# Low part of g on GpSimd, key grams one slot earlier, one-piece inverse steps and gate weights in parts, in an attention and two-MoE kernel

## What is computed

```python
k_n = k / (np.linalg.norm(k, axis=-1, keepdims=True) + 1e-06)
for t in range(S):
    y[:, :, t] = einsum('bhd,bhde->bhe', q[:, :, t], state)
    v_old = einsum('bhde,bhd->bhe', state, k_n[:, :, t])
    state = state + beta[:, :, t] * outer(k_n[:, :, t], v[:, :, t] - v_old)
h = x @ w_in                       # x: y as 3072 x 384
x2 = maximum(0.01 * h, h) @ w_out
logits = x2 @ w_gate + modality_bias[modality_id]
e = argmax(logits)                 # gate_w: softmax(logits)[e]
out = gate_w * (maximum(x2 @ w1[e], 0) @ w2[e])
```

## Time and profile before

| | |
|---|---|
| median of 3 runs | 1023.89 us (1022.36 to 1029.06) |
| profiled execution | 1023.64 us |
| its span | 1021.9 us |
| mean granted clock of PE | 0.951 |
| PE, DVE, ACT, POOL busy | 932.1, 554.3, 351.7, 87.8 us |

### The profile page before, as it was taken

One profiled execution on the slowest core, in us unless ns is written; L12 is line 12 of the kernel. 1 busy time (PEld: TensorE's weight loads), 2 busy tenths in 40 slices (PEclk: granted clock), 3 DMA queues, 4 the chain that ended last, 5 costly groups with the idle time before them and its releaser, 6 DMA issues.

```text
span 1021.9 us, 26857 instructions
## 1 busy us (share of the span) xinstructions
PE 932.1 (91%) x10524; PEld 832.1 (81%) x10525; DVE 554.3 (54%) x1577; ACT 351.7 (34%) x608; POOL 87.8 (9%) x100
## 2 busy tenths in 40 slices
PE   4897699999999999999999999999988999999972
PEld 4896588878888889888888888888877898888962
DVE  5936795389626983498428862334562333333341
ACT  4255234542534343433444242332511222212230
POOL 1000000000020000100010001001021212212211
PEclk8659899999999999999999999999998999999996
DMA  9803181235223440345143411317132111111122
GB/s 161 283 2 73 36 159 57 72 87 88 56 47 89 95 80 26 87 103 94 26 87 81 86 30 29 98 38 202 40 112 99 46 31 46 38 39 46 31 78 70
DMA packets 147923, 77.91 MB, mean 76 GB/s; under 512 B 112112, under 2 KB 143856, under 8 KB 147440
## 3 DMA queue, kind: packets, MB, share of 16 engines
q1 hardware_dynamic: 143728, 66.98, 27.9%
q0 software_dynamic: 4096, 9.48, 3.0%
HBM read 59.30 MB, written 13.21 MB: 71 GB/s over the span
## 4 chain that ended last, share of the span: by engine, by line
PE 73%; DVE 12%; DMA 4%; ACT 3%; issue 3%; SPq 3%; DVEq 0%; POOL 0%; ACTq 0%; POOLq 0%
PE bank L486 16%; PE bank L471 14%; PE bank L567 10%; PE bank L542 9%; PE bank L430 3%; PE bank L457 2%; PE bank L415 2%; PE bank L454 2%; PE bank L362 2%; SPq L737 2%; PE bank L552 2%; DVE inv_t L1264 2%; DVE inv_tmp L1258 2%; PE bank L504 2%; PE bank L383 1%
## 5 line engine op out<-in xcount | busy, mean ns | idle before, releaser
L486 PE MATMUL bank<-wo_hi,g_hi 128*128 128x392 f32 x384 | 138.8, 361 | 8.3 <-DVE g_lo L1338 5.4
L1011 ACT ACTIVATE g_raw<-bank 128x512 f32<-128x512 f32 x96 | 57.3, 597 | 227.4 <-PE bank L471 225.0
L1333 DVE SCALAR_TENSOR_TENSOR g_raw<-g_raw 128x512 f32<-128x512 f32 x96 | 66.2, 690 | 123.6 <-ACT g_raw L1011 122.8
L471 PE MATMUL bank<-x_hi,wi_hi 128*128 128x512 f32 x288 | 118.2, 411 | 16.1 <-DVE x_lo L1329 12.6
L486 PE MATMUL bank<-wo_hi,g_lo 128*128 128x392 f32 x384 | 132.0, 344 | 0.0
L486 PE MATMUL bank<-wo_lo,g_hi 128*128 128x392 f32 x384 | 131.8, 343 | 0.0
L471 PE MATMUL bank<-x_hi,wi_lo 128*128 128x512 f32 x288 | 113.7, 395 | 0.0
L471 PE MATMUL bank<-x_lo,wi_hi 128*128 128x512 f32 x288 | 113.6, 394 | 0.0
L1018 ACT ACTIVATE g_hi<-g_raw 128x512 fp32r<-128x512 f32 x96 | 60.6, 631 | 105.7 <-DVE g_raw L1333 102.6
L1338 DVE TENSOR_TENSOR g_lo<-g_raw,g_hi 128x512 fp32r<-128x512 f32 x96 | 66.1, 689 | 41.8 <-ACT g_hi L1018 40.9
L486 PEld LDWEIGHTS bank<-wo_hi,g_hi 128*128 128x128 f32 x384 | 72.7, 189 | 14.2 <-issue 6.8
(11 more groups left out here) (211 smaller groups left out, 1664.2 us busy)
## 6 DMA issues: line engine op xcount, KB each, us to landing
wo_lo<-wo_lo_d SPq DMA_DIRECT2D x80, 196.0 KB
w_raw<-in_moe_w SPq DMA_DIRECT2D x6, 1536.0 KB, 8.4
x_rows<-stage SPq DMA_DIRECT2D x6, 770.0 KB
kq_in_rows<-in_k SPq DMA_DIRECT2D x6, 768.0 KB, 5.4
k_raw<-in_k SPq DMA_DIRECT2D x24, 192.0 KB, 4.6
vals<-in_v SPq DMA_DIRECT2D x24, 192.0 KB, 4.7
kq_in_rows<-in_q SPq DMA_DIRECT2D x6, 768.0 KB, 7.8
x_raw<-y_t SPq DMA_DIRECT2D x36, 96.0 KB, 2.5
```

Source lines behind the costliest of these rows:

```text
L471: mm = pe.matmul(bank[0][:], a[:, m, P * f:P * f + P], x[:, m, :], start=(m == 0 and x is x_hi and a is wi_hi), stop=(m == KT - 1 and a is ...
L486: mm = pe.matmul(acc[i][:, 0:DX], g[f % 2][:, P * i:P * i + P], w, start=(f == 0 and k == 0), stop=(f == FT - 1 and k == 2))
L1011: act.activation(g_raw[f % 2][:], bank[0][:], ACT.Copy).then_inc(s.hs_ev, 1)
L1333: dve.scalar_tensor_tensor(out=g_raw[f % 2][:], in0=g_raw[f % 2][:], scalar=0.01, in1=g_raw[f % 2][:], op0=ALU.mult, op1=ALU.max).then_inc ...
```

## The change

- `g_lo` is made by POOL instead of DVE in slices f = 0 to 5 and 13 to 15 of a tile (not the very first slice, not in the last tile, and 13 to 15 not in the last two): the slots that hold inverse steps. Two semaphores count the two makers.
- The key transposes all stand at f = 8, the four grams at f = 9 and 10, `norm` at 11, `scale_gram` and the first steps at 12: one slot sooner. The steps end at f = 3 instead of 4.
- An inverse step is one product and one addition instead of two of each; each waits for the one before it.
- The gate weights are made in parts 0 to 8 at (-1, 4), 9 and 10 at (-1, 12), and 11 to 15 at (-1, 13), ahead of the first `up`. The buffers `wo_t` move from x_raw's place to one that overlaps no_token, stage and g_hi; ACT waits for `list_out` before its first copy, and SP no longer waits for the gate products before it loads x. `rest_gate_weights` moves behind `split_x(0)`.
- POOL walks the slots too; its clearing of `inv_t` stands at f = 5, its scatters at f = 9.

```diff
-INV_AT = {13: (0, 5), 14: (5, 9), 15: (9, 13), 0: (13, 17), 1: (17, 21), 2: (21, 25), 3: (25, 30), 4: (30, INV)}
+INV_AT = {12: (0, 4), 13: (4, 9), 14: (9, 12), 15: (12, 16), 0: (16, 20), 1: (20, 24), 2: (24, 28), 3: (28, INV)}
...
-        wo_t = [same_place(f"wo_t{i}", [P, KT, P], sb.at + 4 * DM * i, F32) for i in range(2)]
...
+        wo_t = [same_place(f"wo_t{i}", [P, KT, P], sb.at + at, F32) for i, at in enumerate((2560, 6144))]
...
+        def g_on_pool(n, f):
+
+            return n <= TT - 2 and f < 6 and n + f > 0 or n <= TT - 3 and f >= 13
...
-                pe.wait_ge(s.g_rdy, j + 1)
+                pe.wait_ge(*g_count(n, f))
...
                 if n == -1 and f == 13:
+                    gate_weights(11, FT)
                     up(0, 0)
...
                 if n == -1 and f == 4:
-                    gate_weights()
+                    gate_weights(0, 9)
+                if n == -1 and f == 12:
+                    gate_weights(9, 11)
...
                     if f == 8:
-                        keys_t(n + 2, 0)
-                        keys_t(n + 2, 1)
+                        for m in range(4):
+                            keys_t(n + 2, m)
                     if f == 9:
-                        keys_t(n + 2, 2)
-                        keys_t(n + 2, 3)
+                        gram_k(n + 2, 0)
+                        gram_k(n + 2, 1)
                     if f == 10:
-                        gram_k(n + 2, 1)
-                    if f == 11:
+                        gram_k(n + 2, 2)
                         gram_k(n + 2, 3)
...
-                if n == -1 and f == 10:
-                    sp.wait_ge(s.wx_mm, FT)
...
+            def rest_g(n, f):
+                pool.wait_ge(s.gh_ev, FT * n + f + 1)
+                pool.tensor_tensor(g_lo[f % 2][:], g_raw[f % 2][:], g_hi[f % 2][:].bitcast(F32), ALU.subtract).then_inc(s.g_rdy_p, 1)
...
-            def gate_weights():
-                for f in range(FT):
+            def gate_weights(first, end):
+                if first == 0:
+                    act.wait_ge(s.list_out, 16)
+                for f in range(first, end):
...
+                made = counted(dve.tensor_tensor(
+                    tmp, inv_a[:, j, j + 1:].unsqueeze(2).broadcast_to([P, rows, cols]),
+                    inv_t[:, j, 0:cols].unsqueeze(1).broadcast_to([P, rows, cols]), ALU.mult))
+                dve.wait_ge(s.inv_ch, made)
+                rows_t = inv_t[:, j + 1:, 0:cols]
+                counted(dve.tensor_tensor(rows_t, rows_t, tmp, ALU.add))
```

More of the change, by code:

```diff
@@ L170, in build @@
         inv_t = sb("inv_t", [P, BLK, BLK])
-        inv_tmp = [sb(f"inv_tmp{i}", [P, BLK * BLK // 4]) for i in range(2)]
+        inv_tmp = sb("inv_tmp", [P, BLK * BLK // 4])
         u_sb = sb("u_sb", [P, GROUPS, HD])
@@ L328, in is_set, with g_count @@
             return 0 <= t < SETS
+        def g_on_pool(n, f):
+            return n <= TT - 2 and f < 6 and n + f > 0 or n <= TT - 3 and f >= 13
+        def g_count(n, f):
+            pool = g_on_pool(n, f)
+            done = sum(1 for m in range(n + 1) for e in range(f + 1 if m == n else FT) if g_on_pool(m, e) == pool)
+            return (s.g_rdy_p if pool else s.g_rdy_d), done
         def slots():
@@ L488, in down @@
                 mm.then_inc(s.l2_mm, 1)
-            def gate_weights():
-                pe.wait_ge(s.misc_in, 16 * 6)
-                for f in range(FT + 1):
-                    if f < FT:
+            def gate_weights(first, end):
+                if first == 0:
+                    pe.wait_ge(s.misc_in, 16 * 6)
+                for f in range(first, end + 1):
+                    if f < end:
                         if f % 4 == 0:
@@ L500, in gate_weights @@
                         mm.then_inc(s.wt_mm, 1)
-                    if f:
+                    if f > first:
                         pe.wait_ge(s.wt_ev, f)
@@ L899, in gather, with slot @@
                     ap=ids[x.par][:, 0:1], axis=0), bounds_check=last_token, oob_is_err=False).then_inc(xb_in[x.par], 16)
[L901 to L907, removed]
+            def rest_g(n, f):
+                pool.wait_ge(s.gh_ev, FT * n + f + 1)
+                pool.tensor_tensor(g_lo[f % 2][:], g_raw[f % 2][:], g_hi[f % 2][:].bitcast(F32), ALU.subtract).then_inc(s.g_rdy_p, 1)
+            def slot(n, f):
+                if n >= 0 and f < FT - 1 and g_on_pool(n, f + 1):
+                    rest_g(n, f + 1)
+                if f == 5 and is_set(n + 2) and n >= -1:
+                    pool.wait_ge(s.tt_ready, n + 2)
+                    pool.memset(inv_t[:], 0.0).then_inc(s.tm_zero, 1)
+                if f == 9 and 1 <= n < TT - 1:
+                    if n == 1:
+                        pool.wait_ge(s.list_out, 16)
+                    scatter_ids(n - 1)
+                if f == FT - 1 and 0 <= n < TT - 1 and g_on_pool(n + 1, 0):
+                    rest_g(n + 1, 0)
+            for n, f in slots():
+                slot(n, f)
             pool.wait_ge(s.x_rdy, TT)
@@ L1248, in inverse @@
                 rows, cols = BLK - 1 - j, j + 1
-                cut = (rows + 1) // 2
-                runs = [(a, b) for a, b in ((0, cut), (cut, rows)) if a < b]
-                tmp = inv_tmp[j % 2][:, 0:rows * cols].rearrange("p (r c) -> p r c", c=cols)
+                tmp = inv_tmp[:, 0:rows * cols].rearrange("p (r c) -> p r c", c=cols)
                 if j == 0:
@@ L1254, in inverse @@
                 else:
[L1255 to L1266, removed]
+                    dve.wait_ge(s.inv_ch, steps[0])
+                made = counted(dve.tensor_tensor(
[4 more added lines that the diff above has]
+                counted(dve.tensor_tensor(rows_t, rows_t, tmp, ALU.add))
             def inverse_out(t):
@@ L1337, in rest_g @@
                 dve.wait_ge(s.gh_ev, FT * n + f + 1)
-                dve.tensor_tensor(g_lo[f % 2][:], g_raw[f % 2][:], g_hi[f % 2][:].bitcast(F32), ALU.subtract).then_inc(s.g_rdy, 1)
+                dve.tensor_tensor(g_lo[f % 2][:], g_raw[f % 2][:], g_hi[f % 2][:].bitcast(F32), ALU.subtract).then_inc(s.g_rdy_d, 1)
             routed = [0]
@@ L1523, in slot @@
                     mask_q(n + 2, 0)
-                if ff and f < FT - 1:
+                if ff and f < FT - 1 and not g_on_pool(n, f + 1):
                     rest_g(n, f + 1)
```

44 lines of the change are left out of this document (21 added, 23 removed).

## The result

The changed kernel takes 1031.07 us (median of 17 runs, 1027.05 to 1036.15), the one before beside it 1023.01 (17 runs, 1013.59 to 1029.06): ratio 1.0099 [1.0078, 1.012]. The forecast was 1026.3: the measured median lies above its own range of 1022 to 1030, inside the outer one of 1013 to 1036, and the step up is 8.1 us where 2.7 were forecast. The profiled execution of the changed kernel took 1027.05 us, span 1025.3, the lowest of its runs: 3.4 us of span over before's 1021.9 can be traced, the other 4.7 of the medians' difference can't. The same two kernels were timed twice more: 1.0090 [1.0057, 1.0123] and 1.001 [0.9981, 1.004].

What follows compares the result with a forecast made beforehand. PE was taken to bound the kernel, with DVE pacing 106 to 150 us. From 1023.64 us, +0.8 (merge of set 1), +1.6 (tiles 1 to 4) and +0.3 (key transposes) gave +2.7: 1026.3; own range 1022 to 1030, outer 1013 to 1036.

Steps and rivals of the forecast that it cites:

- rival D: Whole kernel: the Pool step takes 1.63 us and holds DVE, tiles about +3 us each, total 1039 us; chance 0.13.
- Gate weights, first part: Prologue: ACT waits for the list's DMA, first product at 43.9 us, merge of set 0 at 59.3, 5.5 us sooner.
- From there to the first tile: Prologue after set 0's merge: five gate parts at half clock put the first up pass at 108.2 us, 1.9 us late.
- 106 to 150: Stretch paced by DVE: tr ends 2.9 us earlier without Pool's cost; with Pool, merge of set 1 moves by +0.8 us.
- What a Pool g_lo costs: Each g_lo on POOL: 1.25 us in place of 0.69 on DVE, and 0.9 us taken from DVE beside it.
- the signs of being wrong: Up pass before 105 us, DVE's steps stretched a microsecond per slot, or PE's pauses from 150 to 735 above 25 us.
- Rival C: Whole kernel: DVE is held for the whole of each Pool step, +5.6 us in sum, 1029 us; chance 0.20.
- Tiles 1 to 4: Tile starts 1.4 us later, pauses for tr at merges gone (-1.1): +0.4 a tile, +1.6; key transposes add +0.3.
- the scatters move to f=9 and Pool is free there: Slot f=9 of the tiles: moving POOL's scatters there was taken to change nothing.
- the 25 that would have refuted it: Sign of being wrong: PE's pauses between 150 and 735 us adding up to more than 25 us, against 18.3 before.
- A: Prologue: the list does not hold ACT, later gate parts run at full clock, gate weights pay, about 1014 us; chance 0.10.
- B: One-piece steps and Pool cost nothing: stretch 106 to 150 -1 us, tiles -0.5 each, total 1021 us; chance 0.12.

Runs made afterwards that it cites:

- e8_gate_only: The kernel before with only the gate weights made in parts (buffers moved, ACT waiting for the list), against the kernel before: 1025.41 us, 1.0038.
- e1: The changed kernel with every g_lo back on DVE, timed against the kernel before: 1019.59 us, ratio 1.0012.
- e4_dve_two: The changed kernel with g_lo back on DVE and inverse steps in two pieces, timed against the kernel before: 1017.42 us, ratio 0.9983.
- e2_two_piece: The changed kernel with inverse steps in two pieces and two buffers, timed against the kernel before: 1017.24 us, 0.9979; in a later set 1018.10, 0.9977.
- f4_pool_only: The kernel before with only g_lo moved to POOL in the changed kernel's slots, with POOL's clearing and scatters, against the kernel before: 1015.24 us, 0.9931.
- e6_before_again: The kernel before, unchanged, timed and profiled again as its own variant against the kernel before: 1022.37 us, ratio 1.0015.

## Why the prediction was right, and where not

The first result, +8.1 us, is right in direction and inside the outer range, but by luck: most of it comes with the pauses, which the prediction did not have, and the range was that wide for rival D, which did not come. Without the pauses the change is worth -0.4 us, no change that the runs can tell. By its own steps:
- **Gate weights, first part**: right. First product 43.73 (43.9), merge of set 0 at 59.09 (59.3).
- **From there to the first tile**: right in mechanism, 0.5 off in size: 107.70 for 108.2. x_lo ended at 102.9, not 104.5; the five parts at half clock set the date, as the step said. Of 12.7 us taken out nothing arrived, and parts alone cost 0.4% (e8_gate_only).
- **106 to 150**: right. The merge of set 1 starts at 150.29 without a wait; the kernel before's started at 149.37: +0.9 for +0.8. DVE's `tr` was not what set it: it ended at 149.4 as before's did with the earlier trace rows (149.3), where the sum had it 0.7 later, and the merge followed PE's own chain. And the 0.9 doesn't reach the end: tile 1 waits for x_lo in both, 1.47 instead of 2.52 us, and its second up pass starts at 231.71 in both.
- **What a Pool g_lo costs**: 1.30 us in the median for 1.25, and about 0.8 us taken from DVE for 0.9 (34 us over 41), near the microsecond that was one of the signs of being wrong. Rival C's mechanism, the whole step held, is right where an inverse step starts just behind POOL's; its price was not reached.
- **Tiles 1 to 4**: PE's pauses for POOL's g_lo at f = 0 are 1.97, 1.24, 1.20 and 1.25 us, inside the 1 to 2, and none stands before the merges. In the first profile the tiles took 439.1 us from 231.71 to 670.80, 4.1 more than before's 435.0, for +1.9. **The step that failed** is the one that closes this part, "the scatters move to f=9 and Pool is free there", priced at nothing. They start 6.4 us later against DVE's g_lo of that slot, behind the copy of gram 1, and the grams have come to stand beside the last of them; and on occasions PE, ACT and SP stand still around them, PE for 5.3 us instead of 2.8 in this part, and the products beside them come late as well. A second price was missing altogether: a pause of 1 to 2 us can drop PE's clock to 0.50 behind it, 1.4 to 1.7 us each, twice in the changed kernel's tiles and once in before's. Both prices also fall in the kernel before. Without them its tiles would be near 430.8 us by estimate (435.0 less 2.8 less 1.4), and the changed kernel's near 428.9 (430.4 in the profile without pauses, less 1.5 for its one slow stretch): not longer, where +1.9 was forecast. The waits at f = 0 grew from 1.3 to 5.7 us in four tiles, 1.1 a tile for 1.4, and the 4.4 for `tr` went as forecast, so the two cancel.
- Without these occasions the sum, +2.7, stands against -0.4 in the medians and a ratio of 1.001 [0.9981, 1.004]: inside the forecast's own range, with the other sign; that interval, -1.9 to +4.1 us, does not tell +2.7 from nothing. PE's pauses from 150 to 735 sum to 18.75 us (18.3 before), far from the 25 that would have refuted it.
- **Rivals.** A fell (the list held ACT, the parts ran at 0.50). B, at -2.6 us, lies just outside that interval, and it was wrong on one piece: two pieces are 2.8 us faster (1018.10 against 1020.88). D did not come: POOL's step is 1.30, not 1.63.

Why then is POOL's part worth 0.7% in the kernel before and nothing in the changed one (e1: 1.0012, whole change 1.001)? Estimated over two sets, e4_dve_two less e8_gate_only (0.9983 against 1.0038), the early grams are worth about as much, and e2_two_piece with both is no faster than e4_dve_two with one (1017.24 and 1017.42). Both relieve DVE ahead of `tr`, and the pause there can be removed only once. This is argued from the waits; no run has the early grams alone. What is left over is the bill: one piece 2.8 us, gate weights in parts 3.4 (1025.41 against 1022.01). With f4's -6.0 they sum to +0.2, for -0.4 measured.

| part | measured against | change |
|---|---|---|
| g_lo on POOL, alone | before | -0.7% [0.9896, 0.9966] |
| gate weights in parts, alone | before | +0.4% [1.0008, 1.0068] |
| one-piece steps | changed with two pieces, one set | +2.8 us |
| list behind the weights' loads | changed with the list first, one set | +2.4 us |
| early grams | no run alone | about -0.5%, estimated |

## What to carry to other kernels

Cut a change into its parts and time them alone against the kernel before: here the one good part was hidden behind two that cost, and probably a third that did the same job. Two instructions in place of four save fixed costs only if they needn't wait for one another: the dependent ones had 0.195 us against 0.08, and lost. Before a difference of 1% is explained, time and profile the same program on a second occasion; and look where indirect DMAs stand beside runs of short matmuls. Whoever moves work in one engine's list moves what stands behind it: here a copy put into slot f = 9 pushed the scatters of another engine back by 6 us.

## What the hardware showed that I had not expected

- The same program, changed in nothing, took 1029.87 and 1020.88 us in two sets on one chip; the slower one has pauses without a releaser around POOL's scatters on three engines at once. Their cause is open.
- A POOL subtraction of 128x512 takes 1.26 us at the least and up to 2.01 (f4_pool_only), which fits DVE's two-input instructions coming first; DVE's busy time rises by more than the 0.69 that it is spared.
- PE's granted clock fell to 0.50 behind pauses as short as 1.1 us (merges of e8_gate_only at 264.84 and 376.24, and of before at 590.34), though not behind all such pauses: the other three of before's kept 1.00, and so did all four in e6_before_again.
